# Attention with a squared ReLU and a mixture of experts on one core: TensorE's loops nested by batch, the first batch's z work and the routing steps moved, and constant products added at three places

## What is computed

```python
B, S, D = 8, 3072, 256; d_qk = 64
scores = (1.0 / S) * np.matmul(z, z.transpose(0, 2, 1))
attn = np.maximum(scores, 0.0) ** 2
x = (u * np.matmul(attn, v)).reshape(B * S, D)
logits = x @ w_gate                           # E = 8 experts
expert_idx = argmax(logits, axis=1)
gate_w = softmax(logits)[expert_idx]
for i in range(N):                            # tokens in order, capacity 768 each
    if counts[expert_idx[i]] < capacity:
        disp[expert_idx[i], counts[...]] = x[i]; keep[i] = True; counts[...] += 1
h = maximum(einsum('ecd,edf->ecf', disp, w1), 0.0)      # F = 1024
y = einsum('ecf,efd->ecd', h, w2)
out[i] = gate_w[i] * y[expert_idx[i], pos[i]] if keep[i] else 0
```

## Time and profile before

| | us |
|---|---|
| device time, median of 3 executions | 922.24 |
| lowest and highest of them | 921.02, 922.54 |
| the profiled execution's own time | 922.82 |
| its span | 921.0 |
| PE busy in the span | 878.7 |
| DVE busy | 633.7 |
| ACT busy | 600.2 |
| POOL busy | 121.0 |

### The profile page before, as it was taken

The page is one execution under the profiler, slowest core; times in us unless marked ns, Lnnn a source line. Parts: engine busy times, 40 slices in busy tenths (PEclk is TensorE's granted clock), DMA queues, the critical chain, the costliest instruction groups (busy, mean ns, idle before and its releaser), DMA issues.

```text
span 921.0 us, 22938 instructions
## 1 busy us (share of the span) xinstructions
PE 878.7 (95%) x7503; PEld 696.5 (76%) x7504; DVE 633.7 (69%) x1361; ACT 600.2 (65%) x911; POOL 121.0 (13%) x120
## 2 busy tenths in 40 slices
PE   3999899999999999999999999999699999999995
PEld 1787687788888888888888888888477777777774
DVE  6876667877877988879877877687345564656430
ACT  6877686777877778887887787688244344434421
POOL 0001001101101101101110110110112112121212
PEclk9899999999999999999999999999799999999998
DMA  9954409505504650100100000600624245325100
GB/s 267 211 173 160 159 13 318 199 8 170 171 23 148 192 169 17 34 17 17 34 23 11 34 27 19 184 23 17 122 77 112 69 141 160 91 86 143 51 17 34
DMA packets 110663, 90.78 MB, mean 99 GB/s; under 512 B 46909, under 2 KB 105482, under 8 KB 110640
## 3 DMA queue, kind: packets, MB, share of 16 engines
q1 hardware_dynamic: 105744, 77.84, 29.9%
q0 software_dynamic: 4896, 12.64, 3.8%
HBM read 40.03 MB, written 44.93 MB: 92 GB/s over the span
## 4 chain that ended last, share of the span: by engine, by line
PE 87%; DVE 6%; issue 3%; DMA 2%; ACT 1%; POOLq 1%; POOL 0%; DVEq 0%; SPq 0%
PE Sc L736 14%; PE O L622 14%; PE O L624 14%; PE O L626 14%; PE Sc L600 7%; PE Sc L601 7%; PE O L757 5%; PE O L759 5%; PE O L761 5%; PE M L671 1%; DMA disp<-xrow,slot 1%; PE M L576 1%; DVE attn_hi L887 1%; PE M L654 1%; DMA rawz<-in_z 1%
## 5 line engine op out<-in xcount | busy, mean ns | idle before, releaser
L622 PE MATMUL O<-vS,attn_hi 128*128 128x256 f16 x1332 | 364.8, 274 | 0.7 <-DVE ubuf L937 0.7
L626 PE MATMUL O<-vS,attn_lo 128*128 128x256 f16 x1332 | 364.8, 274 | 0.0
L624 PE MATMUL O<-vS,attn_hi 128*128 128x256 f16 x1332 | 364.8, 274 | 0.0
L430 ACT ACTIVATE Sc<-Sc 128x768 f32<-128x768 f32 x224 | 178.6, 797 | 77.6 <-PE Sc L601 67.6
L893 DVE TENSOR_TENSOR attn_lo<-attn,attn_hi 128x768 f16<-128x768 f32 x224 | 214.7, 958 | 7.7
L434 ACT ACTIVATE attn<-Sc 128x768 f32<-128x768 f32 x224 | 181.5, 810 | 7.1
L600 PE MATMUL Sc<-zP 128*128 (+1 forms) x450 | 147.8, 329 | 7.6 <-ACT attn L434 3.3
L887 DVE CAST attn_hi<-attn 128x768 f16<-128x768 f32 x224 | 125.1, 558 | 41.3 <-ACT attn L434 33.3
L622 PEld LDWEIGHTS O<-vS,attn_hi 128*128 128x128 f16 x1332 | 130.7, 98 | 27.4 <-DVE ubuf L937 1.1
L624 PEld LDWEIGHTS O<-vS,attn_hi 128*128 128x128 f16 x1332 | 130.8, 98 | 26.0 <-issue 0.2
L601 PE MATMUL Sc<-zQ,zP 128*128 (+1 forms) x450 | 147.8, 329 | 0.0
(11 more groups left out here) (137 smaller groups left out, 830.9 us busy)
## 6 DMA issues: line engine op xcount, KB each, us to landing
out<-empty SPq DMA_DIRECT2D x8, 3072.0 KB
wraw<-in_moe_w SPq DMA_DIRECT2D x16, 1024.0 KB, 7.7
rawv<-in_v SPq DMA_DIRECT2D x16, 768.0 KB, 8.2
ubuf<-in_u SPq DMA_DIRECT2D x19, 384.0 KB, 3.2
disp<-empty SPq DMA_DIRECT2D x8, 774.0 KB, 16.8
rawz<-in_z SPq DMA_DIRECT2D x3, 768.0 KB, 6.1
disp<-xrow,slot POOLq DMA_INDIRECT x54, 3.1
rawz<-in_z SPq DMA_DIRECT2D x2, 384.0 KB, 4.5
```

Source lines behind the costliest of these rows:

```text
L430: act.activation(pair, pair, ACT.Relu).then_inc(s["relu_done"], 1)
L622: nc.tensor.matmul(o_part(t), hi, v[:, 0:D], start=c == 0 and j == 0 and t % 2 == 0, stop=False, skip_group_check=True)
L624: nc.tensor.matmul(o_part(t), hi, v[:, D:2 * D], start=False, stop=False, skip_group_check=True)
L626: ins = nc.tensor.matmul(o_part(t), lo, v[:, 0:D], start=False, stop=c == PAIRS - 1 and j == 1, skip_group_check=True)
```

## The change

- PE's one loop with an If/Else becomes an outer loop over two batches with two inner loops, one for each copy of the body; the exit on the flag also zeroes the loops' ends.
- The peeled start splits all four slices of z and copies out two of them ahead of v's scale, slice 2 behind the second low part of v and slice 3 at pair 2, all copies on DVE; ACT's `keys_out` is gone. PE transposes slices 0, 1 and 2 ahead of the peeled group and slice 3 behind its pair 2.
- Of the routing chain, the scale moves ahead of DVE's splits of pair 2, the rows' low half from pair 1 to pair 0, the transposes from (2, 0) to (1, 2), the copy of the low transposes from ACT to DVE, the logits from pair 3 to (2, 1), the exponential and all of DVE's routing to pair 2. The counts stay at (3, 1).
- The flag is read after pair 4 (END_AT = 4).
- `turn_over` issues products of constants (128 columns, into a part of a PSUM bank that nothing reads): 60 ahead of the first keys, 72 when PE leaves the attention, 64 behind PE's wait for `attention_over`.

The diff, cut to its core:

```diff
-            def keys_out(q):
...
-                        if peeled and c // PSLICE < SLICES - 2 and c % PSLICE == 1:
-                            keys_out(c // PSLICE + 2)
...
-                            for h in range(2):
-                                act.wait_ge(s["xT_psum"], n * 2 - 1 + h)
-                                act.activation(xT[:, h, :, :]..., Mh[h], ACT.Copy).then_inc(s["xT_ready"], 1)
+                            act.wait_ge(s["xT_psum"], n * 2 - 1)
+                            act.activation(xT[:, 0, :, :]..., Mh[0], ACT.Copy).then_inc(s["xT_ready"], 1)
...
+            def turn_over(times):
+                for _ in range(times):
+                    nc.tensor.matmul(Oa[:, 1, D:D + P], identh[:, :], ones[:, :], start=True, stop=True,
+                                     skip_group_check=True)
+            turn_over(60)
             first_keys(0)
-            pe.wait_ge(s["keys_ready"], 2)
+            first_keys(1)
             scores(0, 0, 0, 0)
             scores(1, 0, 1, 0)
-            first_keys(1)
+            first_keys(2)
             scores(2, 0, 2, 0)
...
-                        if not peeled and c == LOGITS_AT:
...
+                            if not peeled and (c, t) == LOGITS_AT:
...
-                        if peeled and c % PSLICE == 0 and c // PSLICE < SLICES - 2:
-                            first_keys(c // PSLICE + 2)
+                        if peeled and c == LAST_KEYS_AT:
+                            first_keys(SLICES - 1)
...
                 def close():
...
+                    turn_over(72)
+                    for register in (stop0, stop1, stop):
+                        pe.reg_mov(register, 0)
...
-            attention_loop(pe, either_body)
+            body(0, end, 0)
+            pe.reg_mov(stop, NG + 1)
+            pe.reg_mov(low, 1)
+            with pe.Fori(0, stop, 16) as first_of_two:
+                pe.reg_mov(stop0, first_of_two + 8)
+                pe.reg_mov(stop1, first_of_two + 16)
+                with pe.If(first_of_two > NG - 1):
+                    pe.reg_mov(stop0, NG + 1)
+                    pe.reg_mov(stop1, 0)
+                with pe.Fori(low, stop0) as n:
+                    body(nc.s_assert_within(n, 1, NG), end, 0)
+                with pe.If(pe.snap(stop1) > 0):
+                    with pe.Fori(first_of_two + 8, stop1) as n:
+                        body(nc.s_assert_within(n, 8, NG - 1), end, 1)
+                pe.reg_mov(low, first_of_two + 16)
             pe.drain().then_inc(s["pe_over"], 1)
             pe.sem_inc(s["attention_over"], 1)
             pe.wait_ge(s["attention_over"], 5)
+            turn_over(64)
...
             first_z(0)
             first_z(1)
             first_out(0)
+            first_z(2)
+            first_out(1)
+            first_z(3)
             dve.wait_ge(s["vparts0"], SLICES)
             dve.tensor_reduce(mx[:, 1:2], vsum[:, 0:SLICES], AX.X, ALU.add).then_inc(s["vsum0"], 1)
-            first_out(1)
...
             first_v(1)
+            first_out(2)
...
-                        do_hi(K0 + c + 2, c + 2)
-                        do_lo(K0 + c + 2, c + 2)
                         if not peeled and c == RSCALE_AT:
...
+                        do_hi(K0 + c + 2, c + 2)
+                        do_lo(K0 + c + 2, c + 2)
...
+                        if not peeled and c == XT_LO_AT:
+                            dve.wait_ge(s["xT_psum"], n * 2)
+                            dve.tensor_copy(xT[:, 1, :, :]..., Mh[1]).then_inc(s["xT_ready"], 1)
...
-                            first_z(c // PSLICE + 2)
+                        if peeled and c == LAST_KEYS_AT:
+                            first_out(SLICES - 1)
...
-ROWS_LO_AT = 1
-XT_AT = (2, 0)
+ROWS_LO_AT = 0
+XT_AT = (1, 2)
+XT_LO_AT = 1
 XT_OUT_AT = 2
-LOGITS_AT = 3
+LOGITS_AT = (2, 1)
 COUNTS_AT = (3, 1)
-EXP_AT = 3
-ROUTE_AT = (2, 3, 3)
-END_AT = 5
+EXP_AT = 2
+ROUTE_AT = (2, 2, 2)
+END_AT = 4
+LAST_KEYS_AT = 2
```

More of the change, by code:

```diff
@@ L478, in part @@
                         if not peeled and c == XT_OUT_AT:
-                            for h in range(2):
-                                act.wait_ge(s["xT_psum"], n * 2 - 1 + h)
-                                act.activation(xT[:, h, :, :].rearrange("p m n -> p (m n)"), Mh[h], ACT.Copy
-                                               ).then_inc(s["xT_ready"], 1)
+                            act.wait_ge(s["xT_psum"], n * 2 - 1)
+                            act.activation(xT[:, 0, :, :].rearrange("p m n -> p (m n)"), Mh[0], ACT.Copy
+                                           ).then_inc(s["xT_ready"], 1)
                         if not peeled and c == EXP_AT:
@@ L602, in scores @@
                 ins.then_inc(s["scores_ready"], 1)
+            def turn_over(times):
[3 more added lines that the diff above has]
+            turn_over(60)
             first_keys(0)
-            pe.wait_ge(s["keys_ready"], 2)
+            first_keys(1)
             scores(0, 0, 0, 0)
             scores(1, 0, 1, 0)
-            first_keys(1)
+            first_keys(2)
             scores(2, 0, 2, 0)
+            end, stop0, stop1, stop, low = (pe.alloc_register(f"pe_{name}") for name in
+                                            ("end", "stop0", "stop1", "stop", "low"))
             def body(n, end, par):
@@ L673, in part @@
                                     ins.then_inc(s["xT_psum"], 1)
+                            if not peeled and (c, t) == LOGITS_AT:
+                                pe.wait_ge(s["xT_ready"], n * 2)
+                                pe.wait_ge(s["wgs_ready"], 2)
+                                for k in range(TILES):
+                                    for at, (h, m) in enumerate((h, m) for h in range(2) for m in range(DC)):
+                                        ins = nc.tensor.matmul(M[0][:, k * 2 * E:(k + 1) * 2 * E],
+                                                               xT[:, h, m, k * P:(k + 1) * P], wgs[:, m, :],
+                                                               start=at == 0, stop=at == 2 * DC - 1)
+                                ins.then_inc(s["logits_ready"], 1)
                             if not peeled and (c, t) == COUNTS_AT:
@@ L971, in part @@
                             dve.tensor_scalar(tokens, tokens, float(GROUP), None, ALU.add)
-                        if c == PAIRS - 1:
-                            gate_x(n + 1)
-                        do_hi(K0 + c + 2, c + 2)
-                        do_lo(K0 + c + 2, c + 2)
                         if not peeled and c == RSCALE_AT:
@@ L986, in part @@
                             dve.tensor_scalar(rowfac[:, :], rinv[:, :], ginv[:, 0:1], None, ALU.mult)
+                        if c == PAIRS - 1:
+                            gate_x(n + 1)
+                        do_hi(K0 + c + 2, c + 2)
+                        do_lo(K0 + c + 2, c + 2)
                         if not peeled and c == ROWS_LO_AT:
@@ L993, in part @@
                             ins.then_inc(s["rows_lo"], 1)
+                        if not peeled and c == XT_LO_AT:
+                            dve.wait_ge(s["xT_psum"], n * 2)
+                            dve.tensor_copy(xT[:, 1, :, :].rearrange("p m n -> p (m n)"), Mh[1]
+                                            ).then_inc(s["xT_ready"], 1)
                         if peeled and c == GATE_AT[0]:
```

## The result

The changed kernel takes 906.58 us (median of 4, 906.26 to 907.8) against 922.13 us: ratio 0.9836, 95% interval 0.9819 to 0.9853. The forecast was 908.0 us. The profiled execution took 906.26 us, its span is 904.5, so 16.5 us of span are gone.

The account below looks back on a forecast made before the run. PE, busy 95%, was taken to bound the kernel, so only its idle places and low clocks count. -3.2 - 4.6 - 7.2 - 1.0 + 1.4 = -14.6 us gave 908.0 us; own range 904.5 to 911, with rivals 903.5 to 914.5.

Parts of the forecast that it names:

- A, the start: Up to group 1: z's splits ahead of v's scale remove one key slice and both waits for z; -3.2 us.
- the better of the two cases: At the start: clock rising near 24.6 gains 4.2 us; low clock lasting to 28.0 gains 2.5.
- B, the turn: Between groups 1 and 2: PE's 2.9 us "issue" stall and the low clock behind it go; -4.6 us.
- Rival 1: Outer turn at group 16 and passage at group 8 stall like the old jump; 4.6 us for one; chance 0.15.
- C, the groups: Routing chain in the groups: two PE waits, 0.45 us a group, go in 16 groups; -7.2 us.
- The tightest place: PE's pair 4 wants ACT's square of pair 5: margin 0.08 us less some 0.05; no wait taken.
- ACT's v sums: Group 1: too many of them on ACT for it to keep its 0.45 us routing gain.
- the early flag: In the last group: flag comes before PE's queue is through pair 4, so one pair (2.62 us) is never issued.
- Group 4: At its start PE waits 1.25 us because DVE stood for POOL; slots 2.1 us earlier shorten this; -1.0 us.
- D, the end: From flag to experts: slots 2.1 us earlier, 72 products hidden, 64 unhidden and partly at low clock; +1.4 us.
- The prediction's rule on the loop: PE's loop turns: with a 2048-instruction window, inner turns (756) are free, the outer (1,512) near the edge, perhaps one stall.

## Why the prediction was right

Its total was 1.4 us off in the median (2.0 in the profiled span, -16.6 for -14.6), and most terms are near.

- **A, the start: -3.2 forecast, -3.9 in the profile.** PE starts at 21.64, as worked out (21.6), the clock rises at 25.0 and not 28.0, the better of the two cases. Undone, it costs 3.9. The range of 2.5 to 4.2 was too narrow: the start of group 1 varied from 53.4 to 56.5 between executions of kernels with the same start, against 59.2 and 60.3 in those with the old one. So that the one profile came near is in part luck. The sum also priced the old start's low clock (2.6 us) and its waits for z (1.9) side by side. That adds up for the one execution it was read from, but the run with the old start shows that the two trade: with the clock up 2.3 us sooner the wait for slice 2 grew from 0.88 to 1.65 and pair 1 began at the same 28.97. That the 60 products bring nothing held as far as the profiles show; that they moved code was not foreseen.
- **B, the turn: -4.6.** 4.56 when undone, 4.36 alone. In the changed kernel the outer turn costs 0.15 us of queue work. Rival 1, a stall at the outer turn, did not occur in the changed kernel, yet it did in two kernels close to it, for 3.4 to 5.9 us. The chance of 0.15 was too low for a thing that 120 instructions decide. That the changed kernel stands on the free side of it is luck: it owes this to the 60 products, which the prediction held to be worth nothing.
- **C, the groups: 0.45 forecast, 0.47 found**, and every time in the worked chain agrees within 0.1 us (transposes 5.23, logits 7.86, slots 12.63 for 12.62). The tightest place had 0.15 to spare. Two small steps failed. Group 1 kept its gain: it exceeds the plain group by 0.52 us now and by 0.49 before (without the stall at its end), so ACT's v sums took nothing more. And the early flag was said to matter only at the end; it also ended waits at the step from pair 5 to 6 in the early groups, 0.13 us in each of groups 5 to 7 and 0.19 in group 3; with the flag behind pair 5 they came back. Both were missed in the same direction, a good 1 us together.
- **Group 4: -1.0 forecast;** it is 1.77 shorter, of which 0.47 and 0.13 belong above, so about 1.2. It is 33.17 us here, and up to 33.48 in executions of kernels that differ only elsewhere.
- **D, the end: +1.4 forecast, +1.65 found** (3.60 later behind group 18's start, 1.95 back by the high clock). The 72 were hidden, the 64 not; POOL's drain let PE go at 23.9 (24.15 was written). The low clock lasted 5.0 for 4.4.

The runs show free inner turns (756 instructions) in the changed kernel, and an outer turn (1,512) that took 3.66 and 3.36 us in two kernels and 0.21 us in the changed one. The prediction's rule on the loop had foretold free inner turns and an outer one near the edge. Its figure of 2048 is what the Trainium skill's page "Runtime: NRT & Kernel Launch", section "Instruction fetch mechanics", gives as the size of PE's instruction memory. For a taken branch the section speaks of "the current 2-page window", out of which the branch waits for a fetch. The prediction took the one for the other. By an estimate from the 256 instructions that the section gives to each block of a refill, two blocks would be 512. The free inner turns speak against a window of that size. What the exact condition is, the runs don't show.

## What to carry to other kernels

Before filling an idle engine with work that keeps its clock, look on which side of the wait it stands: behind the wait the constant products cost 3.2 us net; ahead of it they cost nothing seen and save the experts the 2.5 us of low clock that they lose without any such products. When an engine's program is large, read the branch durations after every edit, since a wait for code can come and go with instructions that stand outside the loop. And when two steps of one in-order queue are slow, place them at different pairs.

## What the runs showed of the hardware beyond that

- POOL's drain took 82 to 83 ns for each indirect DMA issued since the last drain (54, 48 and 102 of them).
- A taken branch with a packet of the instruction queue inside it took 3.36 to 3.75 us on PE, of which it stood 2.9 to 3.4, and the clock fell behind it in three of four cases (not in the changed kernel without the 60).
- A register load of the flag on PE took 0.93 us in groups 1 to 7 and 0.3 to 0.4 us later.
- A low clock costs nothing where another engine sets the pace: with the old start it rose at 28.0 in one execution and at 25.7 in another, and pair 1 of group 0 began at 28.98 and 28.97.
